# First network's tiles moved by 96 bytes in SBUF, to 352 modulo 512 from the weights

## What is computed

```python
x = attention(q, k, v, alpha)                 # 3072 tokens x 384
for e in range(E):                            # E = 8
    h = np.maximum(x[mask_e] @ w1[e], 0.0)    # 384 -> 1024
    out[mask_e] = gate_w[mask_e, None] * (h @ w2[e])
h = out @ w_in                                # 384 -> 2048
y = np.maximum(0.01 * h, h) @ w_out           # 2048 -> 384
```

## Time and profile before

| | |
|---|---|
| median of 3 runs | 817.96 us (816.58 to 819.44) |
| the profiled execution | 815.64 us, its span 813.8 us |
| TensorE busy | 799.8 us (98%) |
| VectorE / ScalarE / GpSimd busy | 450.8 / 344.6 / 208.0 us |
| line 1721 / 1772 busy on TensorE | 209.8 / 207.2 us |
| line 1674 / 1694 busy on TensorE | 133.7 / 134.8 us |

### The profile page before, as it was taken

The page is one execution under the profiler, slowest core; times in us unless marked ns, Lnnn a source line. Parts: engine busy times, 40 slices in busy tenths (PEclk is TensorE's granted clock), DMA queues, the critical chain, the costliest instruction groups (busy, mean ns, idle before and its releaser), DMA issues.

```text
span 813.8 us, 17577 instructions
## 1 busy us (share of the span) xinstructions
PE 799.8 (98%) x5259; PEld 719.6 (88%) x5260; DVE 450.8 (55%) x705; ACT 344.6 (42%) x643; POOL 208.0 (26%) x278
## 2 busy tenths in 40 slices
PE   7999998999999999999999999999999999999998
PEld 7888877888989989989989898998989898998987
DVE  7899987686567476566565333423433432433332
ACT  3555564566446256444353342333333333324223
POOL 6676722223333343341232021003004001001000
PEclk9999999999999999999999999999999999999999
DMA  9987763767888887897741110201201001000001
GB/s 234 275 249 235 226 224 103 253 208 262 304 281 268 301 271 225 286 298 244 194 57 19 22 39 1 40 1 39 39 0 39 0 0 39 1 1 19 21 1 39
DMA packets 64130, 108.98 MB, mean 134 GB/s; under 512 B 24199, under 2 KB 45747, under 8 KB 64080
## 3 DMA queue, kind: packets, MB, share of 16 engines
q1 hardware_dynamic: 54896, 93.47, 37.4%
q0 software_dynamic: 5888, 14.85, 5.7%
q10 hardware_dynamic: 3296, 0.06, 0.2%
HBM read 78.89 MB, written 30.85 MB: 135 GB/s over the span
## 4 chain that ended last, share of the span: by engine, by line
PE 90%; DVE 3%; DMA 2%; issue 2%; POOL 1%; DVEq 0%; ACT 0%; SPq 0%; ACTq 0%; POOLq 0%
PE bank L1772 25%; PE bank L1721 24%; PE bank L1694 14%; PE bank L1674 14%; PE bank L1516 3%; PE bank L1556 3%; PE bank L1533 2%; PE bank L1564 1%; PE bank L1522 1%; PE bank L1650 1%; DMA xg<-x_rows,isrc 1%; PE bank L1576 1%; DMA qkas<-qka 1%; POOL kt L675 1%; DVE decay L1073 1%
## 5 line engine op out<-in xcount | busy, mean ns | idle before, releaser
L1721 PE MATMUL bank<-yT,wts 128*128 128x512 f32 x864 | 209.8, 395 | 0.3 <-DVE g L1302 0.3
L1772 PE MATMUL bank<-wts,gs 128*128 128x384 f32 x1152 | 207.2, 334 | 0.0
L1772 PEld LDWEIGHTS bank<-wts,gs 128*128 128x128 f32 x1152 | 201.0, 188 | 4.3
L1721 PEld LDWEIGHTS bank<-yT,wts 128*128 128x128 f32 x864 | 161.4, 188 | 35.5 <-DVE g L1302 0.7
L1302 DVE TENSOR_TENSOR g<-bank,small 128x512 f32<-128x512 f32 x96 | 65.9, 687 | 171.9 <-ACT small L929 155.9
L1674 PE MATMUL bank<-wts,gxT 128*128 (+1 forms) x549 | 133.7, 396 | 0.2 <-issue 0.2
L929 ACT ACTIVATE small<-bank 128x512 f32<-128x512 f32 x96 | 57.3, 597 | 164.3 <-PE bank L1721 145.5
L1674 PEld LDWEIGHTS bank<-wts,gxT 128*128 128x128 f32 x549 | 100.8, 188 | 21.3 <-issue 1.1
L1483 DVE TENSOR_TENSOR gs<-g,gs 128x512 fp32r<-128x512 f32 x96 | 66.5, 693 | 66.7 <-ACT gs L1034 64.2
L1034 ACT ACTIVATE gs<-g 128x512 fp32r<-128x512 f32 x96 | 60.7, 632 | 83.6 <-DVE g L1302 76.5
L774 POOL DMA_INDIRECT out<-os,tokens x20 | 19.7, 986 | 283.7 <-ACT os L1023 279.2
(11 more groups left out here) (179 smaller groups left out, 779.8 us busy)
## 6 DMA issues: line engine op xcount, KB each, us to landing
raw<-weights SPq DMA_DIRECT2D x60, 512.0 KB
hidden_rows<-hs SPq DMA_DIRECT2D x29, 512.0 KB
hds<-hidden_rows SPq DMA_DIRECT2D x29, 512.0 KB
qkas<-qka SPq DMA_DIRECT2D x20, 675.5 KB, 5.4
vs<-v SPq DMA_DIRECT2D x24, 192.0 KB, 4.3
x_rows<-xs SPq DMA_DIRECT2D x24, 192.0 KB, 3.9
yl<-y_rows SPq DMA_DIRECT2D x20, 192.0 KB
qkas<-qka SPq DMA_DIRECT2D x4, 227.5 KB, 6.1
```

The source lines that it names most:

```text
L1721: m = pe.matmul(gps[f % 2][:, :], wts[:, 0, w_part, n:n + P], yT[:, 1 - u, y_part, k], start=(k == 0 and (w_part, y_part) == (0, 0)), stop ...
L1772: m = pe.matmul(ops[tt], gs[:, f % 4, g_part, tt * P:(tt + 1) * P], wts[:, 1, w_part, f * D:(f + 1) * D], start=(f == 0 and (g_part, w_par ...
```

## The change

The diff puts gaps between the tiles of the two networks, so that chosen tiles begin at 352 modulo 512 bytes from the start of `wts`. No instruction, wait or order is changed.

```diff
+    LINE, FROM_W1, TO_W_IN, FROM_W2 = 512, 352, 352, 352
...
+            def seat(by):
+
+                here = (nc.sbuf_base + 31) // 32 * 32
+                gap = (wts_at + by - here) % LINE
+                if gap:
+                    sb(f"gap{here}", [P, gap // 4])
+
+            seat(FROM_W1)
             xg_at = (nc.sbuf_base + 31) // 32 * 32
             xg = sb("xg", [P, 2, D])
...
             yf = sb("yf", [P, 2, GT])
+            seat(TO_W_IN)
             yT_at = (nc.sbuf_base + 31) // 32 * 32
             yT = sb("yT", [P, 2, 2, KD, GT], F32R)
...
+            seat(FROM_W2)
             os_at = (nc.sbuf_base + 31) // 32 * 32
             os_ = sb("os", [P, 2, TG, D])
...
-            gs = nc.alloc_sbuf_tensor_at("gs", [P, 4, 2, GT], F32R, offset=hs_at)
-            assert hs_at == xg_at + 2 * D * 4 + 4 * D * 4 and 4 * GT * 4 <= hs_at - xg_at and 8 * GT == 4 * F
+            gs = nc.alloc_sbuf_tensor_at("gs", [P, 4, 2, GT], F32R, offset=hs_at - 96)
+            assert hs_at == xg_at + 2 * D * 4 + 4 * D * 4 and 4 * GT * 4 <= hs_at - 96 - xg_at and 8 * GT == 4 * F
```

## The result

The changed kernel takes 818.75 us (median of 22 runs, 816.23 to 822.22); the kernel before, with 22 runs on the same chips, 816.40 us. The ratio is 1.0031, 95% interval 1.0020 to 1.0042: **2.4 us slower**, where 1.1 us faster was forecast. (The 817.96 of the first three runs was high; with more runs before stands at 816.4.) The profiled execution's span is 816.3 us against 813.8.

What follows compares the result with a forecast made beforehand. TensorE, almost never idle, bounds the kernel through matmul spacing. From 817.96 us, 0.3 (even blocks) and 0.8 (turned rows) come off, all else nil: 1.1 us faster. Range 814.6 to 819.8 us.

Steps and rivals of the forecast that it cites:

- What bounds the kernel: Both networks: TensorE is hardly ever idle, so time is the number of matmuls times their spacing.
- Even blocks' second product: Line 1694, hT_even from 256 to 352: 14 even blocks each get into step 0.02 us sooner, 0.3 us gained.
- Turned rows: Line 1674, gxT loaded at 352: 512-column blocks keep step from the start, 0.04 us each over 23 blocks, 0.8 us gained.
- Rival (b): Line 1674: offset 352 is bad for 512 columns, 0.06 us more a block, +1.1 us net, 819.1; chance 0.12.
- (c): Line 1674: as (b), but every matmul held some 11 ns over the clean 227, +2.9 us, 820.9; chance 0.06.
- (a): Whole kernel: addresses don't matter, gain nil, 817.96 us; chance 0.2.
- (d): Line 1674: the first spacing after the transposes shrinks too, 2.0 us more gained, -3.1, 814.9; chance 0.06.
- What lies ahead of 188 us counts for nothing: Seven earlier first-network blocks: changes vanish in TensorE's wait for a 6.92 us gather landing at 188.3; size nil.
- The three held to be nothing: Second network's matmul spacing, transposes (line 1650, at most 0.2 us either way) and DMAs before 395 us: each counted as nil.
- The modulus: All tiles: only the address offset modulo 512 bytes can matter, since pieces 512 or 1536 bytes apart repeat one duration.

Runs made afterwards that it cites:

- The tables: Offsets of loaded and streamed operands stepped behind the last matmul of the kernel before, other engines idle; only spacings read, 24 matmuls of 512 columns taking 5.70 to 5.87 us.
- gxT alone: Against the kernel before, only gxT moved to 352 modulo 512 from the weights, other tiles as they were; ratio 1.0025, 2.0 us slower.
- all but gxT: Against the kernel before, xg, hs and hT_even moved to 352 modulo 512, gxT kept at 256; ratio 0.9995, no difference.

## Why the prediction was wrong

**What bounds the kernel** was right: TensorE without idle time, and only the spacing of matmuls counts. Nothing but spacings changed, and what followed from them ahead of 188 us.

**Even blocks' second product** was right in size: 4.19 to 4.17 in the even blocks of the stretch without idle time, 12 x 0.02 us; a late one lost 0.07 (last section). gxT alone leaves it at 4.35 from first start to last end, and all but gxT gives 4.33.

**Turned rows** is the step that failed. The trace of before had a comparison of 256 and 352 only for 384 columns (line 1694), where both settle to one spacing. I carried it over to 512 columns as "keeps step from the start". The tables show that the two lengths have different good and bad places, and that 96 modulo 256 is harmless for 384 and the worst for 512. In place of 0.8 us gained it cost 23 x 0.08 = 1.8 us; the stretch with gxT alone moved is 1.9 us longer.

**Rival (b)** named this mechanism and was given 0.12. The only 512-column product at 352 was line 1721, and its 233 ns, never settling, was the better witness, of the same length of stream. I set it aside because there the other operand lies at 352. The tables bear that out in part: with the difference of the addresses deciding, yT at 352 stands for a loaded operand at 160, not at 96. That both of these are slow (5.84 and 5.86) is luck for this rival. Its price was a little low: 0.06 a block over the present, 0.08 measured (397 against 389 ns in the middle, 8 ns where 6 were taken), and so was what it was multiplied with, below. (c) put 11 ns on each and was too high. (a), that addresses don't matter, is refuted by the tables. (d), a shorter first spacing, did not come: the longest duration of a run's first matmuls is 492 ns, where it was 491.

**"What lies ahead of 188 us counts for nothing"** failed too. A wait for a DMA covers only what doesn't also delay the DMA's issue. The gather was issued 0.40 us later, 0.30 of it by the network's own slower blocks. With the 0.25 that this gather took longer, which may be chance, that is 0.54 us of the 2.5.

**The three held to be nothing** held: the second network (209.8 and 207.3 us busy), the transposes (middle duration 272 ns before and after) and the DMAs, since with hs and xg at 352 and gxT at 256 the ratio is 0.9995. That doesn't test the estimate worked out from the Trainium skill (DMA: Bandwidth & Descriptors, How a descriptor splits into AXI transactions), 6% more for rows that start off a 256-byte boundary. The program puts hs at byte 149888 of its partition before and 149984 after, which is 128 and 224 past such a boundary, so its rows were off one in both kernels.

**The modulus.** I argued that only the offset modulo 512 can matter; it is 256, so the "352" of the change is 96, and the 256 it left was 0. The Trainium skill (SBUF — State Buffer, Who interferes with whom) gives TensorE two independent read ports and says that it never waits on anyone. For other engines the tables agree: the slow places cost the same with all of them idle. For its own two reads they don't: 24 matmuls take 5.70 to 5.87 us by their offset alone, and 5.49 when the stream reads one column.

**The range** (814.6 to 819.8) held the 818.75, by way of a level for before that was 1.6 us too high; the sign was wrong.

## What to carry to other kernels

Where TensorE is never idle, look at the settled duration of each product, one by one. The same shape at two values (389 and 394 here) was a place in memory and not work, and the better one costs only a gap of some bytes. A comparison of addresses holds for the length of stream that it was made with; measure a table of offsets once, behind the last instruction of a kernel, for each length, before moving a tile. And look at the product behind the one that is moved, since it can lose part of what the first gains (4.32 to 4.35 here).

## What the runs showed that was not expected

- The difference of loaded and streamed start address modulo 256 bytes sets the time of 24 matmuls of 512 float32 columns to between 5.70 and 5.87 us, almost 3%.
- The best places tried are 0 and 240 modulo 256 for 512 columns (5.70 to 5.74, and 5.71), next 192 (5.75), while 248 takes 5.84; for 384 columns most places give 4.41 to 4.44, and 128 and 160 give 4.48.
- A run can also stay in a slow step at a place where it usually settles. After the change the last even block took 4.40, those between 160 and 400 us 4.33, in TensorE's timeline:

```profile
397.99 4.33 PE L1705 MATMUL bank<-wts,hT_even 128*128 x24
...
411.29 4.40 PE L1705 MATMUL bank<-wts,hT_even 128*128 x24
```

What sends it there is open. It comes behind a product of the second network, not behind one of the first; but the same block took 4.33 before, and 4.33 in the three other kernels that have hT_even at 352.
